# Attention, routing and experts: routing steps on other slots, the last attention pair turned in two pieces, most first weights fetched behind the gather

## The reference

```python
# 1. attention: B, H, S, D = 4, 8, 576, 64, a causal window of 128, ALiBi slopes
scores = scale * q @ k.T + bias      # masked outside of 0 <= rel < 128
attn = softmax(scores) @ v           # x: 2304 tokens x 512
# 2. experts by capacity: E = 8, cap = 2304 / 8 = 288, F = 1024
logits = x @ w_gate
for idx in argsort(-logits.flatten()):      # best pairs of token and expert first
    if token is free and expert has room: assign
out[mask_e] = relu(x[mask_e] @ w1[e]) @ w2[e]
# 3. dense layer: h = x @ w_in (512 x 2048); out = (h * sigmoid(h)) @ w_out
```

## Time and profile before

| | us |
|---|---|
| median of 3 runs | 894.51 (893.71 to 894.56) |
| profiled execution | 896.79 |
| its span in the profile | 895.0 |
| PE busy | 846.1 (95% of the span) |
| DVE busy | 503.9 (56%) |
| ACT busy | 344.8 (39%) |
| POOL busy | 290.1 (32%) |

### The profile page before, as it was taken

One profiled execution on the slowest core, in us unless ns is written; L12 is line 12 of the kernel. 1 busy time (PEld: TensorE's weight loads), 2 busy tenths in 40 slices (PEclk: granted clock), 3 DMA queues, 4 the chain that ended last, 5 costly groups with the idle time before them and its releaser, 6 DMA issues.

```text
span 895.0 us, 17483 instructions
## 1 busy us (share of the span) xinstructions
PE 846.1 (95%) x6605; PEld 790.2 (88%) x6605; DVE 503.9 (56%) x1618; ACT 344.8 (39%) x814; POOL 290.1 (32%) x306
## 2 busy tenths in 40 slices
PE   6999999962999999999999999999999999999998
PEld 6999999951998998899899889998998899899996
DVE  6667676757667386466628462666376466632111
ACT  4666666621333432433333233333332433433222
POOL 1333233413124422622432244225322522532223
PEclk9999999965899999999999999999999999999999
DMA  6666666414203121230412040403121240312000
GB/s 154 168 153 158 152 154 156 112 28 121 83 13 121 44 76 37 86 107 13 122 44 76 1 121 1 123 9 122 54 65 55 68 114 5 121 60 61 1 1 35
DMA packets 117252, 71.42 MB, mean 80 GB/s; under 512 B 61616, under 2 KB 103600, under 8 KB 117168
## 3 DMA queue, kind: packets, MB, share of 16 engines
q1 hardware_dynamic: 114192, 60.85, 25.2%
q0 software_dynamic: 2976, 9.44, 3.4%
HBM read 60.83 MB, written 9.44 MB: 79 GB/s over the span
## 4 chain that ended last, share of the span: by engine, by line
PE 65%; DVE 10%; DMA 2%; issue 1%; ACT 1%; POOL 1%; SPq 0%; POOLq 0%; DVEq 0%
PE hp L1148 11%; PE hp L1150 10%; PE hp L1149 10%; PE acc L1218 7%; PE acc L1220 7%; PE acc L1219 7%; PE acc L1148 4%; PE acc L1150 3%; PE acc L1149 3%; PE rt L1102 2%; DVE test L1360 2%; DVE h_raw L1561 1%; DMA rows<-x_rows,tokens 1%; DVE wa_l L1498 1%; DMA wa_raw<-in_moe_w_dram 1%
## 5 line engine op out<-in xcount | busy, mean ns | idle before, releaser
L1078 POOL TENSOR_TENSOR h_l<-h_raw,h_h 128x256 fp32r<-128x256 f32 (+1 forms) x128 | 103.6, 809 | 268.2 <-ACT h_h L1315 268.0
L1148 PE MATMUL hp<-xy_h,res_h 128*128 128x256 f32 (+1 forms) x512 | 154.6, 302 | 2.3 <-DVE h_raw L1561 2.3
L1561 DVE TENSOR_TENSOR h_raw<-hp,gate 128x256 f32<-128x256 f32 (+1 forms) x128 | 58.3, 456 | 171.1 <-ACT gate L1307 170.1
L1149 PE MATMUL hp<-xy_l,res_h 128*128 128x256 f32 (+1 forms) x512 | 151.4, 296 | 0.0
L1150 PE MATMUL hp<-xy_h,res_l 128*128 128x256 f32 (+1 forms) x512 | 151.3, 295 | 0.0
L1064 POOL TENSOR_TENSOR wb_l<-wb_raw,wb_h 128x512 fp32r<-128x512 f32 x64 | 86.5, 1353 | 139.6 <-ACT wb_h L1261 139.4
L1307 ACT ACTIVATE gate<-hp 128x256 f32<-128x256 f32 (+1 forms) x128 | 52.4, 409 | 171.0 <-PE hp L1150 170.0
L1218 PE MATMUL acc<-res_h,h_h 128*128 128x512 f32 x288 | 116.7, 405 | 0.0
L1220 PE MATMUL acc<-res_h,h_l 128*128 128x512 f32 x288 | 113.6, 395 | 0.0
L1219 PE MATMUL acc<-res_l,h_h 128*128 128x512 f32 x288 | 113.5, 394 | 0.0
L1148 PEld LDWEIGHTS hp<-xy_h,res_h 128*128 128x128 f32 x512 | 96.6, 189 | 8.5 <-DVE h_raw L1561 4.9
(11 more groups left out here) (214 smaller groups left out, 1754.3 us busy)
## 6 DMA issues: line engine op xcount, KB each, us to landing
wa_raw<-in_moe_w_dram SPq DMA_DIRECT2D x64, 256.0 KB, 2.9
wb_raw<-in_moe_w_dram SPq DMA_DIRECT2D x64, 256.0 KB, 3.1
q_rows<-in_q_dram SPq DMA_DIRECT2D x32, 128.0 KB, 3.8
k_rows<-in_k_dram SPq DMA_DIRECT2D x32, 128.0 KB, 3.0
v_rows<-in_v_dram SPq DMA_DIRECT2D x32, 128.0 KB, 2.4
stage<-in_moe_w_in_dram SPq DMA_DIRECT2D x8, 512.0 KB, 4.5
x_rows<-x_rows_sb SPq DMA_DIRECT2D x16, 256.0 KB, 4.2
stage<-in_moe_w_out_dram SPq DMA_DIRECT2D x8, 512.0 KB, 4.6
```

Source lines behind the costliest of these rows:

```text
L1078: pool.tensor_tensor(h_l[:, cols], h_raw[:, cols], h_h[:, cols].bitcast(FP32), ALU.subtract).then_inc(g_low, 1)
L1148: nc.tensor.matmul(out_, weights_h, cols_h, start=start, stop=False)
L1149: nc.tensor.matmul(out_, weights_h, cols_l, start=False, stop=False)
L1561: nc.vector.tensor_tensor(h_raw[:, h_cols(s, f)], hp[(A_NO[s, f] - 1) % 2][:, 0:width], gate[:, 0:width], ALU.mult).then_inc(g_done, 1)
```

## The change

It has four parts. (1) Setup and all steps but step 4 are done at other slots. (2) The last pair is turned in two pieces: tiles 0 to 2 ahead of the last `weighted_values`, and their logits ahead of the turning of tiles 3 and 4; its main copy goes from DVE to ACT. (3) Expert 0's compares are made of 14 and 6 tiles instead of 10 and 10. (4) Of the first eight weight loads only a0 and a1 are issued ahead of the gather; the others wait for a mark that POOL sets behind it, and their conversions move from ahead of the products to the first slots.

```diff
+def main_tiles(g):
+    return TB - 1 if g + 1 < NG else TB - 2
+def logits_at(g):
+    return P * (TB - main_tiles(g))
...
-            def turn_x(g):
+            def turn_x_main(g):
...
                 to = bank("x", g)
-                pe.wait_ge(norm_done, tiles_of_pair(g))
-                for t in range(TB - 1):
+                pe.wait_ge(norm_done, tiles_of_pair(g) if g + 1 < NG else TILES_TO[NS - 2])
+                for t in range(main_tiles(g)):
...
+            def turn_x_end(g):
+                c = slice(P * (g % PAIRS), P * (g % PAIRS + 1))
                 to = bank("e", g)
-                nc.tensor.transpose(to[:, 0:P], x_rows[:, TB - 1, c], ident[:]).then_inc(turned, 1)
-            def gate_logits(g):
-                to = m_ps[TURN_NO["e", g] % 2]
+                pe.wait_ge(norm_done, tiles_of_pair(g))
+                for n, t in enumerate(range(main_tiles(g), TB)):
+                    last = nc.tensor.transpose(to[:, P * n:P * (n + 1)], x_rows[:, t, c], ident[:])
+                last.then_inc(turned, 1)
+            def gate_logits(g, tiles):
+                to, o = m_ps[TURN_NO["e", g] % 2], logits_at(g)
                 pe.wait_ge(wg_loaded, 16)
-                pe.wait_ge(x_taken, g + 1)
-                pe.wait_ge(e_taken, g + 1)
-                for t in range(TB):
-                    last = nc.tensor.matmul(to[:, LG + E * t:LG + E * (t + 1)], xT[:, P * t:P * (t + 1)],
+                if tiles.start == 0:
+                    pe.wait_ge(x_taken, g + 1)
+                if tiles.stop == TB:
+                    pe.wait_ge(e_taken, g + 1)
+                for t in range(tiles.start, tiles.stop):
+                    last = nc.tensor.matmul(to[:, o + E * t:o + E * (t + 1)], xT[:, P * t:P * (t + 1)],
                                             wg[:, g % PAIRS, :], start=True, stop=True)
-                last.then_inc(lg_done, 1)
+                if tiles.stop == TB:
+                    last.then_inc(lg_done, 1)
...
                 if kind == 2 and g >= 1:
-                    turn_x(g - 1)
+                    turn_x_main(g - 1)
+                    turn_x_end(g - 1)
                 if kind == 3 and g >= 1:
-                    gate_logits(g - 1)
+                    gate_logits(g - 1, slice(0, TB))
+            turn_x_main(NG - 1)
             weighted_values(NS - 1)
-            turn_x(NG - 1)
-            gate_logits(NG - 1)
+            bank("e", NG - 1)
+            gate_logits(NG - 1, slice(0, main_tiles(NG - 1)))
+            turn_x_end(NG - 1)
+            gate_logits(NG - 1, slice(main_tiles(NG - 1), TB))
...
                     act.wait_ge(lg_done, g)
-                nc.scalar.activation(xT[:, full:TB * P], m_ps[n % 2][:, 0:P], ACT.Copy).then_inc(e_taken, 1)
+                w = P * main_tiles(g)
+                nc.scalar.activation(xT[:, w:TB * P], m_ps[n % 2][:, 0:TB * P - w], ACT.Copy).then_inc(e_taken, 1)
+            def copy_x_last(g):
+                n = TURN_NO["x", g]
+                w = P * main_tiles(g)
+                act.wait_ge(turned, n + 1)
+                act.wait_ge(lg_done, g)
+                nc.scalar.activation(xT[:, 0:w], m_ps[n % 2][:, 0:w], ACT.Copy).then_inc(x_taken, 1)
...
                     copy_q_low(g + 1)
+            copy_x_last(NG - 1)
...
                     dve.wait_ge(lg_added, g)
-                part = m_ps[TURN_NO["e", g] % 2][:, LG:LG + E * TB].rearrange("p (t e) -> p t e", e=E)
+                o = logits_at(g)
+                part = m_ps[TURN_NO["e", g] % 2][:, o:o + E * TB].rearrange("p (t e) -> p t e", e=E)
...
             normalise(NS - 1)
-            copy_x(NG - 1)
...
-SETUP_AT = {FIRST[2 * _j - 2] + 3: _j for _j in range(1, E)}
-HOOK_LIST = {_j: [FIRST[2 * _j - 2] + _n for _n in (8, 9, 12, 13, 16, 17, 21, 22, 24, 25, 28, 31, 33)]
+SETUP_AT = {FIRST[2 * _j - 2] + 2: _j for _j in range(1, E)}
+HOOK_LIST = {_j: [FIRST[2 * _j - 2] + _n for _n in (7, 8, 11, 12, 16, 20, 24, 25, 27, 28, 31, 34, 38)]
...
 BLOCKS = CAP // BLOCK
-SECOND = 512
+AHEAD = 14
+SECOND = 672
...
-LOADS = sorted([(kind, w) for w in range(E * FT1) for kind in "ab"], key=lambda load: load_key(*load))
-SPLIT_A, SPLIT_B = {}, {}
+LOADS = sorted([(kind, w) for w in range(RING, E * FT1) for kind in "ab"], key=lambda load: load_key(*load))
+LOADS = [("a", 0), ("a", 1), ("b", 0), ("a", 2), ("b", 1), ("a", 3), ("b", 2), ("b", 3)] + LOADS
+SPLIT_A, SPLIT_B = {0: [3]}, {0: [0], 1: [1], AT[0, "b", 0]: [2], AT[0, "b", 1]: [3]}
...
                 e = expert[j]
+                if (kind, w) == LOADS[2]:
+                    sp.wait_ge(fetch_sent, 1)
...
             pool.memset(mark[:], 0.0).then_inc(fetch_sent, 1)
-            for w in range(RING):
-                low_b(w)
...
                     pe.wait_ge(half_part, h // 2)
-                    for t in range(NT // 2):
+                    for t in range(AHEAD):
...
-                    for t in range(NT // 2 if j == 0 and h > 0 else 0, NT):
-                        o = KW[j] * t if j > 0 or h == 0 else SECOND + KW[0] * (t - NT // 2)
+                    for t in range(AHEAD if j == 0 and h > 0 else 0, NT):
+                        o = KW[j] * t if j > 0 or h == 0 else SECOND + KW[0] * (t - AHEAD)
...
             nc.scalar.activation(sig_warm[:], ones[:, 0:1], ACT.Sigmoid)
-            for w in range(RING):
-                high_a(w)
-                high_b(w)
+            high_a(0)
+            high_a(1)
...
                 high_x(0, c, acc[c])
+            high_a(2)
...
                 if j == 0:
-                    t = NT // 2
-                    nc.vector.scalar_tensor_tensor(halves[0], rung[:, None, :].to_broadcast([P, t, k]),
-                                                   base[:, 0:1], keys[:, 0:t, None].to_broadcast([P, t, k]),
-                                                   ALU.add, ALU.is_le).then_inc(half_part, 1)
-                    nc.vector.scalar_tensor_tensor(halves[1], rung[:, None, :].to_broadcast([P, t, k]),
-                                                   base[:, 0:1], keys[:, t:NT, None].to_broadcast([P, t, k]),
-                                                   ALU.add, ALU.is_le).then_inc(dve_part, 1)
+                    for piece, tiles, made in ((pieces[0], slice(0, AHEAD), half_part), (pieces[1], slice(AHEAD, NT), dve_part)):
+                        n = tiles.stop - tiles.start
+                        nc.vector.scalar_tensor_tensor(piece, rung[:, None, :].to_broadcast([P, n, k]), base[:, 0:1],
+                                                       keys[:, tiles, None].to_broadcast([P, n, k]),
+                                                       ALU.add, ALU.is_le).then_inc(made, 1)
...
             low_a(2)
-            low_a(3)
```

More of the change, by code:

```diff
@@ L141 @@
 RING_NEG = 3
-LG = P
 def slot_units(s):
@@ L898, in experts @@
         at_least = test[:, 0:NT * KW[1]].rearrange("p (t k) -> p t k", k=KW[1])
-        halves = [test[:, o:o + KW[0] * NT // 2].rearrange("p (t k) -> p t k", k=KW[0]) for o in (0, SECOND)]
+        pieces = [test[:, o:o + KW[0] * n].rearrange("p (t k) -> p t k", k=KW[0])
+                  for o, n in ((0, AHEAD), (SECOND, NT - AHEAD))]
         onehot = test[:, 0:NT * BLOCK].rearrange("p (t k) -> p t k", k=BLOCK)
@@ L1019, in _ @@
             thresholds(0)
-            pool.memset(test[:, KW[0] * NT // 2:SECOND], 0.0).then_inc(rungs_ready, 1)
-            pool.memset(test[:, SECOND + KW[0] * NT // 2:SECOND + KW[0] * (NT // 2 - 1) + P], 0.0
+            pool.memset(test[:, KW[0] * AHEAD:SECOND], 0.0).then_inc(rungs_ready, 1)
+            pool.memset(test[:, SECOND + KW[0] * (NT - AHEAD):SECOND + KW[0] * (NT - AHEAD - 1) + P], 0.0
                         ).then_inc(rungs_ready, 1)
```

## The result

The changed kernel takes 908.52 us (median of 4 runs, 907.8 to 908.96) against 894.53 for the kernel before (4 runs, 893.71 to 895.84): a ratio of 1.0154, 95% interval 1.0137 to 1.0172. Slower, as forecast, but by 14.0 us and not by 2.1; the time lies above the whole range of 892.5 to 903. The profiled execution took 907.8 us, span 906.1.

What follows compares the result with a forecast made beforehand. TensorE was busy 846.1 of 895.0 us, so its gaps mattered, steadily those from late VectorE work. Gone 15.9 and 0.5 of `reached` waits, new 18.5: net +2.1 on the 894.51 median, 896.6 us; range 892.5 to 903.

Steps and rivals of the forecast that it cites:

- a4: First-layer product of a routed expert's tile 4, waiting for tile 2's `h_l` behind setup: 12.1 us in six later cycles.
- The start: Expert 0's first product some 5.5 us earlier: loads 3.3, last attention pair 1.7, 14 and 6 tiles 0.5.
- Step 8: Steps 7 and 8 at slots 25 and 27: `h_raw` delays `digit`, PE waits 0.6 in six cycles, 3.6 in sum.
- Clock: Rival: waits of 2 us cost TensorE its clock; two falls give 902, seven 914; chance 0.13.
- Its price of 2.5 a fall: Clock rival's cost per fall: from a0 to a4, first cycle at low clock 12.1 us, second cycle 9.6.
- The argument against it: Against the clock rival: in later slices, with waits up to 1.3 us, the clock stays at 9 throughout.
- The row that spoke for it: For the clock rival: after 0.86 us idle at attention's end, four transposes take 0.92, about twice their full-clock time.
- The first cycle's wait: At least 0.8 us behind setup, plus 0.9 for each of two POOL splits meeting setup; taken as 2.5.
- POOL: Next expert's gather, later in POOL's queue, ends at 38.8 us, its reader b11 stands at 38.9; 0.3 charged.
- The rival: POOL's queue: `h_l` of tile 11 comes later than chained, b11 waits 0.76 in six cycles: 901 us; chance 0.12.
- The waits that go: Last routing step's waits for `out_tokens`, 8.1 us, and first-layer product's for `h_raw`, 2.3, all go: 10.4.
- The covered splits: Second-layer splits once covered by the gather's time, now by the first three first-layer tiles: nothing, 1 us if cover fails.

Runs made afterwards that it cites:

- busy wait: Changed kernel with unused products into the idle bank `rt` ahead of a4, so TensorE stays busy while waiting: 902.99 us, ratio 1.0083.
- shorter waits without a fall: Changed kernel with `h_l` of tile a2 issued ahead of setup's last two operations: 901.23 us, ratio 1.0074.
- the loads alone: Kernel before with the fourth part alone, weight loads behind the gather and first second-layer tiles split in the first routed stage: 895.99 us, ratio 1.0011.
- setup in slot 2: Kernel before with setup at slot 2 instead of 3 and nothing else changed: 916.43 us, ratio 1.024.
- the slots alone: Kernel before with setup in slot 3 and steps in 7 8 11 12 16 20 23 24 26 27 30 33 37, nothing else: 883.99 us.
- the same slots with parts 2 to 4: Changed kernel with setup in slot 3 and steps in 7 8 11 12 16 20 23 24 26 27 30 33 37: 884.62 us, ratio 0.9874.
- setup in slot 3: Changed kernel with setup back at slot 3, all other parts kept: 890.87 us, ratio 0.9947.

## Why the prediction was wrong

The sign and the places were right; the size failed on the clock and on some smaller terms. By the two traces:

**Right.** The waits of the earlier trace rows are gone but for 0.3 of 10.4. In the six later cycles a4 is late by 1.92, 2.06, 2.30, 2.31, 1.89 and 2.03: 12.5 us against 12.1. The start moved by 5.9 against 5.5; the three kernels that start as before have their first product at 225.15 to 226.33, the nine with parts 2 to 4 at 219.61 to 221.63, means 5.4 apart. Step 8 was right as well: `digit` starts 0.96 behind step 7's product (0.95 forecast), the compare ends 3.46 behind it (3.47), and the step comes 0.56 late in each of six cycles, in sum 3.4 us against 3.6. The list shows 0.40 for it, counted from the product's end.

**Clock, the step that failed.** I gave the rival 0.13 and left it out of the sum. Four falls came. Its price of 2.5 a fall was about right for the first cycle (2.2 by the busy wait; there PE stayed at the lower level from 236.40 to some 241.6) and twice too high for the three later ones (1.2, 1.1 and 1.3). Together they make 5.9 us. The argument against it was that waits up to 1.3 us leave the clock alone, from which nothing follows for waits of 2. The row that spoke for it, the slow transposes behind 0.86 us idle, was the nearer one (0.92 us for four, where the pair before took 0.60; I had called that twice). The experiments show the mechanism from both sides: shorter waits without a fall (901.2 us) and the same lateness without idling (903.0). The Trainium skill ("TensorE: Matmul & The Clock Gate", Part 1) describes a drop after an idle stretch; I read it as sparing a gap of 2 us, and 14 falls behind gaps of 1.8 to 2.4 us in these runs contradict that reading.

**The first cycle's wait.** a4 was forecast 2.5 late and is 3.9 late; the listed wait is 4.4. A third split met setup, and stretching costs 1.1 and not 0.9. The listed wait is larger than the lateness because the clock now rises 4.1 us after the first product and not 5.6, so that a4 was wanted sooner against DVE's work.

**POOL**, 0.3 forecast, 2.5 listed: some 0.46 in each of five cycles and less in the sixth; from start to start b11 costs about 3.8. The rival had it nearly right, with 0.76 a cycle and its margin of 0.1 us. What broke the margin was an issue stretched by a `wa_l` on DVE, which I had only looked for in splits.

**The waits that go**, 10.4 forecast, are worth 13.0 from start to start, 0.2 more for each of 13. I took them from the list, and the new ones from starts.

**The covered splits**, costed at nothing and 1 us "if the cover fails". They cost nearly the whole gain of the loads: 3.4 us in the run of the loads alone, 1.8 of it a wait and the rest a fall of the clock. In the changed kernel this cost is in the first cycle's wait and its fall.

These make +5.9 (clock), +1.4 (first a4), +1.2 (dense stages: -2.6 waits gone, -0.2 step 8, +3.5 POOL, +0.5 the one `h_raw` wait in the list) and -0.4 (start): 8.1 of the 8.9 us by which the profiled execution (907.8) exceeds the one forecast from it (898.9). The rest lies in the routed stages and isn't resolved.

The last 3 us between 896.6 and 908.52 come of the executions that were compared: the profiled one of before was 2.3 above its median, that of after 0.7 below. Part of the 2.3 can be seen. In the profiled execution of before the clock rose 5.6 us after the first product; in the two kernels that start as it does (setup in slot 2, and the slots alone) it rose after 3.4 and 3.9, and the first routed stage of the slots alone is 0.8 us shorter. So the growths of the first stage that are given above against before are some 0.8 too small, an estimate from this one pair.

The prediction's range of the sum has a slip: with all bounds one way it is -1.1 and not -1.6. Nothing hangs on it.

## What to carry to other kernels

Price a wait that is new to a steadily busy TensorE as the wait and a fall of its clock, unless the trace shows one of that length without; shaving 0.3 to 0.6 us off each was worth 7 us here. Take all terms of a sum by one measure, from starts or from the list of waits; here the two differ by 0.2 us a wait. When work is taken off the path at the start, ask which engine is full in the next stage: the loads' earlier start met a late DVE and was worth nothing, and the slots alone did as well as the same slots with parts 2 to 4 (883.99 and 884.62). Of a step on a shared queue, what counts is what it puts in front of the next reader: with the long compare ahead of `h_l` the kernel took 908.52 us, with it behind 890.82, as with setup in slot 3 (890.87).

## What the runs showed of the hardware

In cycles 3 and 5 the clock fell some 1.2 and 0.5 us after PE had resumed; in the first cycle, with 4.4 us idle, inside the wait (mean 0.70 from 234 to 236). None of 10 waits of 1.34 to 1.76 us amid dense products was followed by a fall, and 14 of 16 of 1.80 to 2.38 us were, 0.3 to 2.0 us after PE had resumed. The two without were 1.85 and 2.14 us long, while waits of 1.80 to 1.82 had one in three kernels. So length isn't all of it, and what else decides stays open.

A short DVE operation of setup that meets a POOL `tensor_tensor` isn't slowed in proportion; it ends up to 0.2 us after the other does: 0.17 to 0.33 us become 1.24 to 1.41. DVE operations that read PSUM kept their time beside one (`h_l` 0.46, `h_raw` 0.42, `reached` 0.16). The reverse holds too: POOL's indirect issues took 1.20 and 1.33 us beside a `wa_l`, 0.92 without. The Trainium skill ("SBUF — State Buffer", "SBUF: two separate sides") has the two engines share a port pair that one of them holds for a whole instruction; the stretched rows agree with it.
